# Relative-position attention and a dense mixture of experts on one core: eight places for bias rows, their first load behind a later store, another order of pass 0's first four steps, bias blocks over later positions

## The reference, cut to what matters

```python
# B, H, S, D = 2, 8, 576, 64 ; N = B*S = 1152 tokens, E = 4 experts, 512 -> 1024 -> 512, all float32
scores = scale * q @ k.T                                    # per batch and head, 576 x 576
x = log1p(|i - j|) / log1p(max(i, 1))
bias[h, i, j] = relu(x * w1 + b1) @ w2[:, h]                # 32 hidden units, 8 heads, the same for both batches
attn = exp(s - max(s)); attn = attn / (sum(attn) + 1e-9)    # s = scores + bias
x = (attn @ v) as [1152, 512]
p = domain_probs / (sum(domain_probs) + 1e-9)
out = sum over e of p[:, e] * (relu(x @ w1[e]) @ w2[e])     # every expert on every token
```

## Time and profile before

| | |
|---|---|
| median of three runs | 618.24 us |
| the profiled execution, and its span | 619.06 us, 617.2 us |
| PE busy | 581.0 us (94%) |
| DVE, ACT, POOL busy | 296.1, 262.7, 119.7 us |
| mean granted TensorE clock | 0.98 of full |

### The profile page before, as it was taken

How to read it: one execution, slowest core, us unless ns; L and a number is a source line. 1 busy time by engine, 2 the same in 40 slices (tenths; PEclk the granted TensorE clock), 3 DMA queues, 4 the chain that set the end, 5 groups by cost and what they waited for, 6 DMA issues and landing times.

```text
span 617.2 us, 9758 instructions
## 1 busy us (share of the span) xinstructions
PE 581.0 (94%) x3864; PEld 468.1 (76%) x3864; DVE 296.1 (48%) x608; ACT 262.7 (43%) x506; POOL 119.7 (19%) x176
## 2 busy tenths in 40 slices
PE   3857998979999999999999999999999999999997
PEld 1325666636678878878888788998899889889986
DVE  6925776679535543365334633362254226224511
ACT  4645666487626644365344643252045015303400
POOL 5124888100001135231342311000000000000000
PEclk9966999989999999999999999999999999999999
DMA  4773665187372723465152311341233014122201
GB/s 149 200 276 116 192 193 147 69 237 218 116 235 65 236 84 89 111 184 160 36 171 87 119 35 70 103 137 34 69 84 121 35 35 139 66 69 60 79 35 51
DMA packets 60654, 72.72 MB, mean 118 GB/s; under 512 B 23232, under 2 KB 39872, under 8 KB 60608
## 3 DMA queue, kind: packets, MB, share of 16 engines
q1 hardware_dynamic: 60416, 72.08, 38.4%
q10 hardware_dynamic: 192, 0.01, 0.0%
HBM read 59.10 MB, written 12.98 MB: 117 GB/s over the span
## 4 chain that ended last, share of the span: by engine, by line
PE 84%; DMA 4%; ACT 4%; DVE 3%; issue 2%; POOL 2%; SPq 0%; ACTq 0%; DVEq 0%; POOLq 0%
PE m_bank L1095 12%; PE scores L1078 11%; PE x_bank L1095 11%; PE m_bank L1078 10%; PE scores L1095 10%; PE x_bank L1078 9%; PE turn L1029 5%; PE scores L1000 4%; PE scores L1058 4%; PE scores L968 3%; DMA bias_scratch<-rows 3%; PE x_bank L1058 3%; PE turn L968 2%; PE turn L1033 1%; DVE hidden L679 1%
## 5 line engine op out<-in xcount | busy, mean ns | idle before, releaser
L627 POOL TENSOR_SCALAR probs<-probs,recip 128x576 f32<-128x576 f32 x72 | 53.2, 749 | 234.0 <-DVE recip L714 233.7
L730 DVE TENSOR_TENSOR w_lo<-w_raw,w_hi 128x1024 fp32r<-128x1024 f32 x64 | 80.4, 1256 | 21.1 <-ACT w_hi L885 21.1
L699 DVE CUSTOM_DVE_ANT_0 probs<-scores,bias 128x576 f32<-128x576 f32 x72 | 51.9, 754 | 49.5 <-PE scores L1000 37.6
L869 ACT COPY probs_t<-turn 128x512 f32<-128x512 f32 (+2 forms) x80 | 42.4, 551 | 68.8 <-PE turn L1029 67.6
L885 ACT CAST w_hi<-w_raw 128x1024 fp32r<-128x1024 f32 x64 | 66.6, 1045 | 0.2 <-DMA w_raw<-w_in 0.2
L863 ACT ACTIVATE probs<-probs,neg_max 128x576 f32<-128x576 f32 x72 | 55.4, 772 | 26.6 <-DVE neg_max L699 26.6
L1029 PE MATMUL turn<-ident,probs 128*128 128x128 f32 x288 | 45.2, 285 | 3.4 <-POOL probs L627 3.3
L1078 PE MATMUL scores<-x_hi,w_hi 128*128 128x384 f32 (+2 forms) x148 | 47.8, 323 | 0.0
L1078 PE MATMUL scores<-x_lo,w_hi 128*128 128x384 f32 (+2 forms) x148 | 47.3, 319 | 0.0
L1078 PE MATMUL scores<-x_hi,w_lo 128*128 128x384 f32 (+2 forms) x148 | 47.2, 319 | 0.0
L1078 PE MATMUL m_bank<-x_hi,w_hi 128*128 128x512 f32 (+2 forms) x124 | 44.9, 362 | 0.0
(11 more groups left out here) (138 smaller groups left out, 1256.8 us busy)
## 6 DMA issues: line engine op xcount, KB each, us to landing
w_raw<-w_in SPq DMA_DIRECT2D x64, 512.0 KB, 3.5
qk_raw<-qk_t_in SPq DMA_DIRECT2D x16, 576.0 KB, 4.5
bias<-bias_scratch SPq DMA_DIRECT2D x16, 576.0 KB, 4.8
bias_scratch<-rows SPq DMA_DIRECT2D x16, 288.0 KB, 5.3
v<-v_in SPq DMA_DIRECT2D x32, 128.0 KB, 3.3
bias_scratch<-probs_t SPq DMA_DIRECT2D x10, 288.0 KB, 3.0
out_dram<-acc SPq DMA_DIRECT2D x8, 256.0 KB, 2.0
bias_scratch<-probs SPq DMA_DIRECT2D x5, 288.0 KB, 3.0
```

The costliest lines, as they stand in the source:

```text
L627: pool.tensor_scalar(tile, tile, recip[:, stat(f, p, j)], 1.0, ALU.mult, ALU.mult).then_inc(normed, 1)
L699: dve.tensor_tensor_reduce(probs_of(f, p, j).rearrange("p (c j) -> p c j", c=2), score_of(f, j)[:, :, 0:HALF], bias_of(f, p, j).rearrange( ...
L730: dve.tensor_tensor(lo, raw, hi.bitcast(F32), ALU.subtract).then_inc(w_lo_out, 1)
L869: act.copy(sub_out(f, p, i), sub_in(n, i)).then_inc(out_act, 1)
```

## The change

- Blocks 0 to 15 have eight places for rows: the four before, and the four tiles of `probs_2`, which hold the probabilities of odd pairs later. `add_bias` of pair 1, half 0, so waits until stores 8 to 15 have landed.
- `load_bias0(0, 0)` is issued behind the store of block 11 instead of that of block 8, and `load_bias0(1, 0)` behind all stores and behind `load_bias0(0, 1)`.
- The first four steps of pass 0 run in the order (0,0), (1,0), (0,1), (1,1). At the fifth step PE takes the turns of step (0,1) ahead of the score step, and product 0 comes one step later (`PRODUCTS_AT`). POOL splits q and k of pairs 3 to 9 one step later.
- Blocks 16 and 17 are summed between the parts that fill the end of pass 0. SP stores them ahead of its loads of chunks 2 and 3. Blocks 18 to 35 are at positions 3 to 11, two each, and pass 1 starts at position 14.
- The first hidden part of `ge` = 4 is taken apart, so that its last quarter alone waits for the end of pass 1.

```diff
-ROW_RING = 4
+ROW_RING = (8, 4)
+STORES = 8
-FIRST_SLOT = 12
+FIRST_SLOT = 14
+ORDER0 = [(0, 0), (1, 0), (0, 1), (1, 1)] + [(p, t) for p in range(2, PAIRS) for t in range(2)]
+PRODUCTS_AT = {5: 0, 6: 1, **{2 * p + 4: p for p in range(2, PAIRS - 1)}}
+BIAS_AT = {pos: (EARLY + 2 * pos - 4, EARLY + 2 * pos - 3) for pos in range(3, 12)}
...
             if n < EARLY:
-                return rows[:, n % ROW_RING, :]
+                return (rows, probs_2)[n // 4 % 2][:, n % 4, :]
...
@@ SP
-                store_rows(0)
-                load_v(0, 0)
-                for n in range(1, EARLY):
+                for n in range(EARLY):
                     store_rows(n)
...
-                    if n == 8:
+                    if n == 11:
                         rows_all_stored(EARLY // 2)
                         load_bias0(0, 0)
-                    if n == 10:
-                        load_raw(3)
-                    if n == 12:
-                        load_bias0(1, 0)
                 rows_all_stored(EARLY)
-                load_bias0(0, 1)
-                load_bias0(1, 1)
+                for m, t in ((0, 1), (1, 0), (1, 1)):
+                    load_bias0(m, t)
...
+                store_rows(EARLY)
+                store_rows(EARLY + 1)
                 load_chunk(2)
                 load_chunk(3)
...
@@ DVE, add_bias
+                        elif p == 1 and j < 2:
+                            for rows_n in range(EARLY - STORES, EARLY):
+                                rows_are_stored(dve, rows_n)
...
@@ ACT, DVE and PE, positions of the experts
-                        if ge == 0 and EARLY + 2 * pos < BLOCKS:
-                            scale_block(EARLY + 2 * pos)
-                            scale_block(EARLY + 2 * pos + 1)
+                        if ge == 0 and pos in BIAS_AT:
+                            for n in BIAS_AT[pos]:
+                                scale_block(n)
...
@@ PE
                 for s in range(STEPS + 1):
+                    if s == LAG + 2:
+                        turns_of_step(*ORDER0[s - LAG])
                     if s < STEPS:
-                        score_step(0, p, t)
+                        score_step(0, *ORDER0[s])
+                    if s >= LAG and s != LAG + 2:
+                        turns_of_step(*ORDER0[s - LAG])
+                    if s in PRODUCTS_AT:
+                        products(0, PRODUCTS_AT[s])
...
                 hidden_part(0, 1, 0, 0, MT - 1)
                 products(0, PAIRS - 1)
+                sum_block(EARLY)
                 hidden_part(0, 2, 0, 0, MT - 1)
+                sum_block(EARLY + 1)
                 pe.wait_ge(x_lo_out, PAIRS)
...
+                pe.wait_ge(x_lo_out, 2 * PAIRS - 2)
+                hidden_part(E, 0, 0, 0, MT - 1)
                 pe.wait_ge(x_lo_out, 2 * PAIRS)
+                hidden_part(E, 0, 0, MT - 1, MT)
```

More of the change, by code:

```diff
@@ L59, with turn_order @@
 SLOTS = 6
-FIRST_SLOT = 12
+FIRST_SLOT = 14
 CHUNK = 1024
+ORDER0 = [(0, 0), (1, 0), (0, 1), (1, 1)] + [(p, t) for p in range(2, PAIRS) for t in range(2)]
+STEP_N = {step: s for s, step in enumerate(ORDER0)}
+PRODUCTS_AT = {5: 0, 6: 1, **{2 * p + 4: p for p in range(2, PAIRS - 1)}}
 def blk(f, p, j):
-    return BLKS[0] * p + j if f == 0 else BLKS[0] * PAIRS + BLKS[1] * p + j
+    return 2 * STEP_N[p, j // 2] + j % 2 if f == 0 else BLKS[0] * PAIRS + BLKS[1] * p + j
+def turn_order():
+    order = []
+    for p, t in ORDER0:
+        order += [(0, p, 2 * t), (0, p, 2 * t + 1)] + [(0, p, 4)] * t
+    return order + [(1, p, i) for p in range(PAIRS) for i in range(TURNS[1])]
+TURN_ORDER = turn_order()
+TURN_N = {turn: n for n, turn in enumerate(TURN_ORDER)}
 def turn_n(f, p, i):
-    return TURNS[0] * p + i if f == 0 else TURNS[0] * PAIRS + TURNS[1] * p + i
+    return TURN_N[f, p, i]
 def inverted(f, p, t):
-    return 2 * p + t + 1 if f == 0 else STEPS + 3 * p + t + 1
+    return STEP_N[p, t] + 1 if f == 0 else STEPS + 3 * p + t + 1
 def place_of(g):
@@ L99, in turn_taken @@
     out, count = [], {True: 0, False: 0}
-    for f in range(2):
-        for _ in range(PAIRS):
-            for i in range(TURNS[f]):
-                on_act = i in ACT_TURNS[f]
-                count[on_act] += 1
-                out.append((on_act, count[on_act]))
+    for f, _, i in TURN_ORDER:
+        on_act = i in ACT_TURNS[f]
+        count[on_act] += 1
+        out.append((on_act, count[on_act]))
     return out
@@ L112, in taken_by @@
 def taken_by(f, p):
-    upto = TAKEN[:turn_n(f, p, TURNS[f] - 1) + 1]
+    upto = TAKEN[:max(turn_n(f, p, i) for i in range(TURNS[f])) + 1]
     return sum(a for a, _ in upto), sum(not a for a, _ in upto)
@@ L233, in attention_and_experts @@
             hidden_sb = sb(early, "hidden", [P, HID_RING, QUADS, S])
-            rows = sb(early, "rows", [P, ROW_RING, S])
+            rows = sb(early, "rows", [P, 4, S])
             probs_2 = sb(early, "probs_2", [P, BLKS[0], S])
@@ L259, in attention_and_experts @@
             sem(s) for s in ("hid_dve", "hid_act", "hid_used", "scaled"))
[L260 removed]
+        rows_stored = [sem(f"rows_stored{r}") for r in range(STORES)]
         cleared = sem("cleared")
```

125 lines of the change are left out of this document (65 added, 60 removed).

## The result

The changed kernel took 622.26 us (median of 6 runs, 620.98 to 624.27), the kernel before, run beside it on the same chip, 617.34 us (6 runs, 615.92 to 618.50): ratio 1.0079, 95% interval [1.0055, 1.0104], some 4.9 us slower. The profiled execution of the changed kernel took 620.98 us, its span 619.2 us, mean granted clock 0.978.

A forecast was written before the change was run, and what follows sets the result against it. It took PE work to bound the kernel except at 36 to 52 us and 121 to 133 us, where PE waits. 619.06 - 4.0 + 7.3 = 622.4 profiled, median 621.5 us; 8 in 10 range 616.4 to 625.2.

The forecast's parts named there:

- Places and stores: Start of pass 0: ACT never waits for stores, last scaling ends at 36.2, last store lands at 42.0, 4.7 us earlier.
- The first steps: Pass 0's reordered steps: scores of step 6 start at 62.3 against 66.31, 4.0 us gained, transfer savings partly given back.
- Positions 0 to 3: Late chunk loads behind stores: PE stands 10.5 us before sum 18; 13.3 added, 6.0 removed, 7.3 us lost.
- Clock: Late wait: clock falls to half behind PE's idle time; loss 7.3 us, against 4.5 with a clock that stays up.
- The rest: Pass 1 and its end: idle may shift 1 us either way, split last hidden part covers its wait; taken as nothing.
- Sum: Whole kernel: 619.06 - 4.0 + 7.3 = 622.4 us for the profiled execution, a median of 621.5 us.
- not slower: Rival on transfers: quicker, pass 0 gains 6.4, chunk loads at 3.4 each make the loss 6.1; median 617.9; chance 0.16.
- Faster: Rival on late chunks: they cost nothing, the 6.0 us of before vanish; median 608.2; chance 0.10.
- Pass 0's start gives nothing: Rival on early steps: clock stays at half through steps 3 to 5, 0.5 of gain left; median 624.9; chance 0.14.

The follow-up runs named there:

- scores_first: Changed kernel with the score matmuls ahead of the turns at the fifth step, as at all other steps: 621.05 us.
- both_first: Changed kernel with chunks 2 and 3 loaded ahead of stores 16 and 17, and hidden tiles of blocks 18 and 19 made ahead of position 0: 615.72 us.
- warm: Changed kernel with 40 matmuls whose result nobody reads, filling PE's idle time before sum 18: 620.99 us.
- early_only: Kernel before with only the early part of the change (eight places, new loads, new order of steps): 615.34 us beside 618.06.
- chunks_first: Changed kernel with chunks 2 and 3 loaded ahead of the stores of blocks 16 and 17: 617.78 us.
- late_only: Kernel before with only the late part of the change (bias blocks 16 and on moved, chunks 2 and 3 behind stores 16 and 17): 625.58 us.
- early_old_steps: Kernel before with eight places and the new order of loads, old order of steps and old late part: 613.56 us beside 617.78.
- best: Early part of early_old_steps, late part of both_first, and at position 3 ACT's bias work ahead of its hidden part and chunk work: 616.89 us.
- places_only: Kernel before with eight places for bias rows instead of four, nothing else: ratio 1.0004.
- tiles_first: Changed kernel with the hidden tiles of blocks 18 and 19 made ahead of position 0's work on ACT and DVE: 618.75 us.

## Why the prediction was right, and where it was off

It said 621.5 us and slower; measured were 622.26, and slower. By its steps:

- **Places and stores.** ACT waits for no store, as said; the last scaling ended at 34.9 (36.2 said). The loads behind the last store were issued at 40.8, where 42.0 was said. But I priced places and loads as one; with the moved loads SP goes on, and the places alone are worth nothing.
- **The first steps.** Score step 6 started at 62.2 (62.3 said), and that is luck: DVE's third step started at 44.93 (45.9 said) and product 0 at 59.0 (60.0 said), each 1.0 early, but product 0 ran at half clock and took 0.9 longer than the 2.31 in the working. Nor did the last store set these steps in the changed kernel's trace. DVE's first and third step (start, us, what, [idle before <- releaser]):

```profile
37.81 0.76 DVE L723 CUSTOM_DVE_ANT_0 probs<-scores,bias 128x576 f32<-128x576 f32 x1 [5.70 <-DMA bias<-bias_scratch]
44.93 0.76 DVE L723 CUSTOM_DVE_ANT_0 probs<-scores,bias 128x576 f32<-128x576 f32 x1 [1.82 <-PE scores L1031]
```

  The first bias load, for which the working has no term, took 6.56 us from 31.23 on, and the second and third step waited for scores at half clock behind it (so also in scores_first, both_first and warm). In early_only and chunks_first it was the last store and the load behind it, as said. The two paths are close: in the changed kernel the load for (0,1) landed some 0.3 us before the third step began. As a difference the term is mis-sized: it was 4.0 us, the median of early_only says 2.7. One trace each was the wrong measure. Product 7 starts between 110.22 and 112.28 in the seven kernels with the new early part (mean 111.1), so the changed kernel's trace, the fastest of its six runs, was the earliest of the seven; with the old early part it starts at 114.64 and 114.95, and at 111.26 in the fast run of late_only. "Partly given back" was right; the runs add that the new order of steps did the giving back (1.5 us), while I had counted it as part of the gain.
- **Positions 0 to 3.** Every link came where it was put: chunk 2 behind store 17 (4.03 us to land, 4.4 said), chunk 4 (3.57, 3.6 said), PE idle 9.65 (10.5 said), two sums at half clock. The hidden part behind them ran in 2.95 us at the full clock; the 0.6 us that I added for it was not there. Term 7.3; late_only measured 7.5, and the marks give (66.04 + 66.25 + 65.59) / 3 = 66.0 against a mean of 59.0 over the six traces with the old late part, so 7.0. That the term fits so well is partly luck. The 13.3 us that I added were 11.4 in the trace (9.65 idle, and 1.7 for the two sums), and of the 6.0 that I took off, 1.67 were half clock, which the second trace of the kernel before doesn't have. From product 7 to the output PE is idle for 9.8 us in the changed kernel and 4.6 in that trace, and busy 1.9 longer: 7.2.
- **Clock.** The prediction put 7.3 - 4.5 = 2.8 us of the late loss on it; warm gives 1.9, with intervals that overlap, and its trace 1.5. What it read from the earlier trace rows held: the engine had been idle for 9.65 us and came back at half clock, and with the idle time filled it did not fall. By the Trainium skill ("TensorE: Matmul & The Clock Gate", Part 1) activity is what releases the throttle, and warm, at a granted clock of 1.00, agrees.
- **The rest.** Taken as nothing; the last column of the table gives 0.1 us, the split last hidden part of pass 1 with it.
- **Sum.** Said: +3.3 us. Measured: +4.9, where the halves by themselves gave -2.7 and +7.5. The forecast difference was 1.6 us short; that the time itself came within 0.8 us is owed to the base, 618.24 in the runs I started from and 617.34 in those beside the changed kernel.

Of the rivals, "not slower" fell on the chunk loads: the last store did land near 40.7, but the two loads took 7.6 us together where it needed 6.8, and the early part gave less than half of its 6.4. "Faster" failed in both of its conditions. "Pass 0's start gives nothing" saw one thing rightly, half clock at product 0, and not its size.

## What to carry to other kernels

A queue that issues in order makes a wait costly by what stands behind it: here more places for the producers were worth nothing while a load that waits stood ahead of their stores, and with that load three stores later and another behind the last store, 4.5 us were gained. When bias work, stores and weight loads share one queue, follow the chain from the last matmul through store and load back to the next matmul before moving any of them; here it was worth 4.8 us whether two stores or two loads of weights stood first. Split a change into its parts before keeping it: this one held a gain of 4.3 us (places, loads, old steps) that its other parts turned into a loss of 4.9.

## What was not expected of the hardware

- The same transfers vary by some microseconds from run to run. The last early store took 5.76 and 7.34 us in the traces of early_only and chunks_first, 5.23 and 6.11 in those of early_old_steps and best, and within each pair the programs are the same up to there. The pair of profiles, one of each kernel, showed 2.0 us (span 617.2 and 619.2) where the medians differ by 4.9.
- The clock's fall is not fixed either. The kernel before, with the same wait of 2.53 us ahead of sum 20, ran sum 21 in 2.15 us in one trace and in 1.18 in the other; early_only ran both sums at half clock behind that same wait, places_only and early_old_steps none. The Trainium skill ("TensorE: Matmul & The Clock Gate", Part 1) says that the monitor's window runs freely of the kernel, so that the same kernel has more or fewer slow matmuls at its start from run to run. These traces agree that it varies, here in the middle of a kernel. Waits of 9.6 us were followed by half clock in all three traces that had one (changed, late_only, scores_first), and so were those of 5.72 and 5.57 us in chunks_first and tiles_first (in the latter the first matmul of 512 columns takes 0.76 us, behind 2.54 us of idle time in both_first 0.47).
